# The second network's first product in seven block products for each pair of token tiles

## What is computed

```python
def _attn_ref(q, k, v):                       # q, k, v: (8, 8, 576, 64)
    q_s = softmax over d of q; k_s = softmax over the sequence of k
    kv = np.einsum('bhsd,bhse->bhde', k_s, v)
    return np.einsum('bhsd,bhde->bhse', q_s, kv)

def _moe_ref(x, w_in, w_out, alpha):          # x (4608, 512), w_in (512, 2048)
    h = x @ w_in
    g = np.maximum(h, 0.0) + alpha * np.minimum(h, 0.0)
    return g @ w_out

def _moe2_ref(x, w_in, w_out, g_ln):          # w_in (512, 1024), w_out (1024, 512)
    h = x @ w_in
    e = np.exp(h - np.max(h, axis=-1, keepdims=True))
    solu = h * e / (np.sum(e, axis=-1, keepdims=True) + 1e-09)
    mu, var = mean and variance of solu over its row
    return ((solu - mu) / np.sqrt(var + 1e-06) * g_ln) @ w_out
```

## Time and profile before

| what | us |
|---|---|
| median of 3 runs | 1226.35 (1226.23 to 1227.88) |
| profiled execution | 1226.08 |
| its span, first to last instruction | 1224.3 |
| PE busy | 1209.1 (99%), 6129 matmuls |
| DVE busy | 818.4 (67%) |
| ACT busy | 508.8 (42%) |
| POOL busy | 206.5 (17%) |

### The profile page before, as it was taken

How to read it: one execution, slowest core, us unless ns; L and a number is a source line. 1 busy time by engine, 2 the same in 40 slices (tenths; PEclk the granted TensorE clock), 3 DMA queues, 4 the chain that set the end, 5 groups by cost and what they waited for, 6 DMA issues and landing times.

```text
span 1224.3 us, 16516 instructions
## 1 busy us (share of the span) xinstructions
PE 1209.1 (99%) x6129; PEld 1002.5 (82%) x6129; DVE 818.4 (67%) x1060; ACT 508.8 (42%) x720; POOL 206.5 (17%) x179
## 2 busy tenths in 40 slices
PE   8899999999999999999999999999999999999998
PEld 7788888888888888888888888897888888888887
DVE  7867677676773577869777697665755565655652
ACT  4444444434443344444344443333543444344442
POOL 5632423223231000000000000021211111111110
PEclk9999999999999999999999999999999999999999
DMA  9798787877855654261552614693544444444432
GB/s 237 218 265 260 231 258 233 251 254 226 269 176 167 241 189 170 93 225 52 171 173 69 225 50 140 203 269 120 169 157 139 147 145 146 147 139 151 137 120 78
DMA packets 208973, 217.52 MB, mean 178 GB/s; under 512 B 63480, under 2 KB 147984, under 8 KB 208784
## 3 DMA queue, kind: packets, MB, share of 16 engines
q1 hardware_dynamic: 204672, 208.30, 53.8%
q0 software_dynamic: 4192, 8.39, 2.3%
q10 hardware_dynamic: 48, 0.01, 0.0%
HBM read 124.84 MB, written 91.81 MB: 177 GB/s over the span
## 4 chain that ended last, share of the span: by engine, by line
PE 95%; DVE 2%; DMA 1%; SPq 1%; issue 0%; ACT 0%; POOL 0%; DVEq 0%; ACTq 0%
PE ps_y L1608 11%; PE ps_y L1610 10%; PE ps_y L1609 10%; PE ps_y L1694 5%; PE ps_y L1696 5%; PE ps_y L1698 5%; PE ps_y L1748 5%; PE ps_y L1746 5%; PE ps_y L1747 5%; PE ps_m L1721 3%; PE ps_m L1696 3%; PE ps_m L1698 3%; PE ps_m L1694 3%; PE ps_h L1726 3%; PE ps_h L1721 3%; PE ps_m L1726 3%
## 5 line engine op out<-in xcount | busy, mean ns | idle before, releaser
L1608 PE MATMUL ps_y<-X,W 128*128 128x512 f32 x576 | 226.7, 394 | 0.0
L1610 PE MATMUL ps_y<-X,W 128*128 128x512 f32 x576 | 224.4, 390 | 0.0
L1609 PE MATMUL ps_y<-X,W 128*128 128x512 f32 x576 | 224.3, 389 | 0.0
L1215 DVE SCALAR_TENSOR_TENSOR gst<-gst,nslope,ps_y 128x512 f32<-128x512 f32 x144 | 105.1, 735 | 129.7 <-ACT gst L863 129.6
L863 ACT ACTIVATE gst<-ps_y 128x512 f32<-128x512 f32 x144 | 85.8, 596 | 236.0 <-PE ps_y L1610 211.7
L1608 PEld LDWEIGHTS ps_y<-X,W 128*128 128x128 f32 x576 | 108.1, 188 | 23.1
L1610 PEld LDWEIGHTS ps_y<-X,W 128*128 128x128 f32 x576 | 108.1, 188 | 22.8
L1609 PEld LDWEIGHTS ps_y<-X,W 128*128 128x128 f32 x576 | 108.1, 188 | 21.9
L1694 PE MATMUL ps_y<-rh,WOc 128*128 128x512 f32 (+1 forms) x320 | 117.8, 368 | 1.3 <-DVE rl L1357 1.3
L1696 PE MATMUL ps_y<-rl,WOc 128*128 128x512 f32 (+1 forms) x320 | 117.7, 368 | 0.0
L1698 PE MATMUL ps_y<-rh,WOc 128*128 128x512 f32 (+1 forms) x320 | 117.7, 368 | 0.0
(11 more groups left out here) (186 smaller groups left out, 2356.8 us busy)
## 6 DMA issues: line engine op xcount, KB each, us to landing
g_scratch<-gst SPq DMA_DIRECT2D x144, 256.0 KB, 3.2
RX<-g_scratch SPq DMA_DIRECT2D x36, 512.0 KB, 3.6
z_scratch<-zb SPq DMA_DIRECT2D x35, 512.0 KB, 2.6
zt<-z_scratch SPq DMA_DIRECT2D x140, 128.0 KB, 2.8
RY<-g_scratch SPq DMA_DIRECT2D x18, 512.0 KB, 4.5
RZ<-g_scratch SPq DMA_DIRECT2D x18, 512.0 KB, 4.3
x2r<-y_scratch SPq DMA_DIRECT2D x36, 256.0 KB, 3.1
KK<-k_dram SPq DMA_DIRECT2D x16, 512.0 KB, 6.9
```

The lines of the kernel that those rows point to most:

```text
L1215: nc.vector.scalar_tensor_tensor(gst[:, n % 3, :], gst[:, n % 3, :], nslope[:, f:f + 1], ps_y[:, f % 4, :], ALU.mult, ALU.add).then_inc(g_ ...
L1608: nc.tensor.matmul(o, W1[:, f, 0, a, :], x[:, 0, a, :], start=(a == 0), stop=False)
L1609: nc.tensor.matmul(o, W1[:, f, 0, a, :], x[:, 1, a, :], start=False, stop=False)
L1610: mm = nc.tensor.matmul(o, W1[:, f, 1, a, :], x[:, 0, a, :], start=False, stop=(a == KT - 1))
```

## The change

The first product of the second network takes its tiles in pairs (period n, tiles t = 0 and 1) and makes h of both in seven block products by the same recursion as the down product: the left operand's blocks are x parts of the two tiles and their sums, the right operand's are blocks and sums of blocks of W_in2. A block is 6 matmuls of 512 columns, a pair has 42.

- The seven x operands are made once for a whole pass of the down product: the four quadrants, and three sums and one further difference that POOL forms from them (`x2_sums`, `x2_lower`). SP stores all seven to `x2_dram`.
- The seven W operands are made in the first stage (`ws_turn`, four differences for each half), 22 pieces instead of 16, four per chunk.
- h is put together in SBUF (`hs`) by ACT (`first_copy`, `h11_copy`) and DVE (`form_u`, `form_v`, `form_22`, `form_12`, `form_21`); maximum, exponential and solu read it there. solu and z are written over e2. The squares go to PSUM.
- `x2_low` on POOL takes the 14 blocks of a pair at once, 128x1792.
- All loops are written out, the first five periods in an order of their own, the rest in a fixed one. The last tile's transposes by PE are gone.

```diff
+        W2c, = place(ATT_AT, ("W2c", [P, 7, 2, 2, TOK], F32R))
+        BLOCK = (m0, m1, ps_h[:, 0, :], ps_h[:, 1, :], m0, m1, ps_h[:, 0, :])
...
@@ sync: after a pass of the down product
+            def store_sums(u):
+                store_x2(u, 1, p1, s1_ok, u + 1, s1_st)
+                store_x2(u, 3, u1, s3_ok, u + 1, s3_st)
+                store_x2(u, 2, c11, s2_ok, u + 1, s2_st)
+            def store_lower(u):
+                store_x2(u, 4, v1, c21_ok, 2 * (u + 1), y21_st)
+                store_x2(u, 5, v1, s4_ok, u + 1, s4_st)
+            def load_x2(n):
...
+                if n >= 2:
+                    sp.wait_ge(x2h_ok, n - 1)
+                    sp.wait_ge(x2l_ok, n - 1)
+                sp.dma_start(x2[n % 2][:, :, :], x2_dram[u, :, :, :, r * P:(r + 1) * P].rearrange("k a p n -> p (k a) n")
+                             ).then_inc(x2_in[n % 2], 16)
@@ gpsimd
+            def x2_sums(u):
+                n = TOK // 2 if u == PAIRS else TOK
+                pool.wait_ge(c12_ok, 2 * (u + 1))
+                pool.wait_ge(y22_st, 16 * (u + 1))
+                nc.gpsimd.tensor_tensor(p1[:, :, 0:n], u1[:, :, 0:n], p1[:, :, 0:n], ALU.add).then_inc(s1_ok, 1)
+                pool.wait_ge(s1_ok, u + 1)
+                pool.wait_ge(c11_ok, u + 1)
+                nc.gpsimd.tensor_tensor(u1[:, :, 0:n], c11[:, :, 0:n], u1[:, :, 0:n], ALU.subtract).then_inc(s3_ok, 1)
+                pool.wait_ge(s3_ok, u + 1)
+                pool.wait_ge(y11_st, 16 * (u + 1))
+                nc.gpsimd.tensor_tensor(c11[:, :, 0:n], p1[:, :, 0:n], c11[:, :, 0:n], ALU.subtract).then_inc(s2_ok, 1)
+            def x2_lower(u):
+                n = TOK // 2 if u == PAIRS else TOK
+                pool.wait_ge(s2_ok, u + 1)
+                pool.wait_ge(y21_st, 16 * (u + 1))
+                nc.gpsimd.tensor_tensor(v1[:, :, 0:n], v1[:, :, 0:n], c11[:, :, 0:n], ALU.subtract).then_inc(s4_ok, 1)
+            def load_w2(n):
+                k, last = 2 * n, min(2 * n + 2, PARTS)
+                pool.wait_ge(b_used, ends(LAST_U, n))
...
+            for u in range(PAIRS):
+                x2_sums(u)
+                x2_lower(u)
             pool.wait_ge(ws_st, 16 * WS)
+            for n in range(4):
+                load_w2(n)
+            x2_low(0)
+            load_wo2(0)
+            load_wo2(1)
+            x2_sums(PAIRS)
+            x2_low(1)
+            x2_lower(PAIRS)
+            x2_low(2)
+            power(0, 0)
+            x2_low(3)
+            power(0, 1)
+            power(1, 0)
+            x2_low(4)
...
+            for n in range(5, PERIODS):
+                power(n - 1, 0)
+                power(n - 1, 1)
+                if n + 1 < PERIODS:
+                    x2_low(n + 1)
@@ scalar
+            for n in range(5, PERIODS):
+                square_tile(n - 1, 1)
+                first_copy(n)
+                out_copy(n - 3, 0)
+                zt_high(n - 2, 0)
+                if n + 1 < PERIODS:
+                    x2_high(n + 1)
+                out_copy(n - 3, 1)
+                zt_high(n - 2, 1)
+                h11_copy(n)
+                exp_tile(n, 0)
+                exp_tile(n, 1)
+                square_tile(n, 0)
@@ vector
+            def form_u(n):
...
+                nc.vector.tensor_tensor(hs[n % 2][0][:, TOK:F2], BLOCK[2], p1c[:, :], ALU.add).then_inc(h_u, 1)
+            def form_v(n):
...
+                nc.vector.tensor_tensor(hs[n % 2][1][:, 0:TOK], BLOCK[3], hs[n % 2][0][:, TOK:F2], ALU.add).then_inc(h_v, 1)
...
+            form_early(0)
+            form_12(0)
+            tile_max(0, 0)
+            form_21(0)
+            tile_max(0, 1)
+            tile_solu(0, 0)
+            form_early(1)
+            tile_solu(0, 1)
+            form_12(1)
+            form_21(1)
+            norm_tile(0, 0)
+            tile_max(1, 0)
+            form_early(2)
+            norm_tile(0, 1)
+            zt_low(0, 0)
+            tile_max(1, 1)
+            tile_solu(1, 0)
+            form_12(2)
+            form_21(2)
+            tile_solu(1, 1)
+            tile_max(2, 0)
+            tile_max(2, 1)
+            zt_low(0, 1)
+            norm_tile(1, 0)
+            form_early(3)
+            norm_tile(1, 1)
+            tile_solu(2, 0)
+            zt_low(1, 0)
+            tile_solu(2, 1)
+            form_12(3)
+            form_21(3)
+            tile_max(3, 0)
+            norm_tile(2, 0)
+            tile_max(3, 1)
+            norm_tile(2, 1)
+            zt_low(1, 1)
+            tile_solu(3, 0)
+            form_early(4)
+            tile_solu(3, 1)
+            norm_tile(3, 0)
+            zt_low(2, 0)
...
+            for n in range(5, PERIODS):
+                norm_tile(n - 1, 0)
+                norm_tile(n - 1, 1)
+                form_early(n)
+                zt_low(n - 2, 0)
+                zt_low(n - 2, 1)
+                form_12(n)
+                tile_max(n, 0)
+                form_21(n)
+                tile_max(n, 1)
+                tile_solu(n, 0)
+                tile_solu(n, 1)
+            n = PERIODS - 1
+            norm_tile(n, 0)
+            norm_tile(n, 1)
+            for t in range(2):
+                zt_low(n - 1, t)
...
@@ tensor
+            def m1_product(n, k):
+                if k == 0:
+                    pe.wait_ge(x2l_ok, n + 1)
...
+                elif k == 1 and n > 0:
+                    pe.wait_ge(h12_ok, n)
...
+                elif k == 5:
+                    pe.wait_ge(h22_ok, n + 1)
...
+                for t in range(2):
+                    begin = t == 0 and not more
+                    nc.tensor.matmul(o, hi[:, 2 * k + t, :], W2c[:, k, 0, t, :], start=begin, stop=False,
+                                     skip_group_check=more)
+                    nc.tensor.matmul(o, hi[:, 2 * k + t, :], W2c[:, k, 1, t, :], start=False, stop=False,
+                                     skip_group_check=more)
+                    mm = nc.tensor.matmul(o, lo[:, 2 * k + t, :], W2c[:, k, 0, t, :], start=False, stop=(t == 1),
+                                          skip_group_check=more)
+            for n in range(PERIODS):
+                for k in range(4):
+                    m1_product(n, k)
+                if n >= 3:
+                    m2_product(n - 3, 1)
+                for k in range(4, PARTS):
+                    m1_product(n, k)
+                if n >= 2:
+                    m2_product(n - 2, 0)
+            m2_product(PERIODS - 3, 1)
+            for n in range(PERIODS - 2, PERIODS):
+                for t in range(2):
+                    m2_product(n, t)
```

More of the change, by code:

```diff
@@ L679, in _ @@
[L679 to L693 removed]
+                    load_x2(0)
@@ L779, in x2_low @@
-            def x2_low(m, r):
-                pool.wait_ge(x2h_ok, 4 * m + r + 1)
-                nc.gpsimd.tensor_tensor(x2l[:, r % 2, :, :], x2[r], x2h[:, r % 2, :, :].bitcast(F32),
-                                        ALU.subtract).then_inc(x2l_ok, 1)
-            def power(m, r):
-                s = r % 2
-                pool.wait_ge(var_ok, 4 * m + r + 1)
-                nc.gpsimd.tensor_tensor(st[:, s, 8:9], st[:, s, 7:8], mhalf[:, :], ALU.pow).then_inc(rstd_ok, 1)
-            def tiles(m, last=False):
-                for r in range(4):
-                    if not (last and r >= 2):
-                        x2_low(m + (r + 2) // 4, (r + 2) % 4)
-                    power(m, r)
@@ L803, in _ @@
+            power(PERIODS - 1, 0)
+            power(PERIODS - 1, 1)
         @block.scalar
@@ L1072, in _ @@
-            exp_tile(0, 3)
-            x2_high(1, 1)
-            square_tile(0, 3)
-            out_copy(0, 0, first=True)
-            tiles(1, second=True)
-            with act.Fori(2, LAST) as m:
-                tiles(m)
-            tiles(LAST, last=True)
-            zt_high(LAST, 2)
-            out_copy(LAST, 1, last=True)
-            zt_high(LAST, 3, by_pe=True)
-            out_copy(LAST, 2, last=True)
-            out_copy(LAST, 3, last=True)
+            first_copy(2)
+            x2_high(3)
@@ new lines, in _ @@
+            exp_tile(1, 0)
+            h11_copy(2)
+            zt_high(0, 0)
+            exp_tile(1, 1)
+            square_tile(1, 0)
+            zt_high(0, 1)
+            square_tile(1, 1)
+            first_copy(3)
+            out_copy(0, 0)
+            x2_high(4)
+            exp_tile(2, 0)
+            exp_tile(2, 1)
+            zt_high(1, 0)
+            out_copy(0, 1)
+            square_tile(2, 0)
+            h11_copy(3)
+            square_tile(2, 1)
+            zt_high(1, 1)
@@ L1475, in zt_low @@
[L1475 to L1488 removed]
+                dve.wait_ge(z_ok, i + 1)
@@ new lines, in norm_tile, with zt_low, form_early @@
+                if n > 0:
+                    dve.wait_ge(zb_st[t], 16 * n)
+                nc.vector.transpose(zb_out[t], zb_in[t]).then_inc(zb_ok, 1)
+            def zt_low(n, t):
+                dve.wait_ge(zh_ok, 2 * n + t + 1)
```

(16 more changed lines are left out.)

760 lines of the change are left out of this document (410 added, 350 removed).

## The result

The changed kernel takes 1243.22 us (median of 4 runs, 1241.06 to 1245.13), the kernel before 1226.29 on the same chip: a ratio of 1.0134, 95% interval 1.0121 to 1.0147. It is slower, as forecast (1239, range 1214 to 1251).

The account below looks back on a forecast made before the run. TensorE was taken to bound the kernel, 95% of the span. Terms -25.5 + 23.0 + 13 + 2 = +12.5 on 1226.08 to 1226.35 gave 1239 us; own range 1226 to 1246, 8 in 10 1214 to 1251.

Parts of the forecast that it names:

- The matmuls removed: Second network: 108 fewer matmuls at 0.227 us, 24.5 us, and the last tile's eight transposes, 1.0 us: -25.5.
- The turns at the down product: GpSimd's sums and VectorE's operations with two SBUF inputs take turns, delaying b_low: +23.0 us, +21 to +26.
- The start of the second network: First pairs: TensorE waits for late forms, x2_low and the first z tiles: +13 us, ends 4 and 17.
- The end: Last period: both last tiles' norms stand ahead of zt_low(16,0), so TensorE waits: +2 us, range 0 to 2.6.
- The first stage: Six more splits and eight differences, 0.7 us each, beside up products: not charged, at most 1 us.
- Sums that are free: Rival, chance 0.14: GpSimd's sums in the down product cost nothing, giving -15 us, 1211.
- A second network without stalls: Rival, chance 0.11: the down product pays, but the second network starts without stalls: -2.5 us, 1224.
- Rival 3: Second network, chance 0.10: x2_low blocks z's scaling every period, 22.0 instead of 20.4 us: +21, 1260.

Follow-up runs that it names:

- pool_reads: Kernel before, plus four GpSimd subtractions of 128x1024 on an unused buffer behind each of passes 1 to 4, nobody waiting: 1247.07 us, ratio 1.0177.
- dve_sums_early_last: Changed kernel, sums of passes 1 to 4 on VectorE, pass 4's late ones early in the last pass, x2_low(0) on VectorE behind the last b_low: 1229.42 us.
- pool_writes: Kernel before, plus GpSimd memsets, which write SBUF and read nothing, four times behind each of passes 1 to 4: 1226.72 us, ratio 1.0001.
- x_low_one_column: Changed kernel, GpSimd's x2_low cut to one of 128 columns from pair 2 on, the other low parts left out: 1242.38 us, ratio 1.0115.
- early_x2_loads: Changed kernel, only queue orders altered around the second network's start and end, with x2 loads earlier: 1243.90 us, ratio 1.0146.
- sums_one_column: Changed kernel, sums of x made for one column of each row only, semaphores and stores kept: 1227.33 us, ratio 1.0002.

## Why the prediction was right

**The matmuls removed** (-25.5). Steady periods are 20.40 us long against 21.76 for two tiles before. The pitch of 0.227 is unchanged. VectorE is busy for 16.7 us of a period where 18.0 was counted.

**The turns at the down product** (+23.0, measured +22.2). The mechanism was the one laid out, and a sum in a free field took the 2.40 that stood in the count. The sizes hold pass by pass too: 5.3 stood for each of three passes, 4.9, 4.9 and 4.6 were measured; 7.1 stood for the short fifth (5.4 + 1.7), 7.5 was measured; the first pass has 0.3, where nothing stood. The brackets alone give less, waits of 2.99, 3.57 and 4.04 in passes 2 to 4, because a pass also holds restarts, the shortest waits and, in pass 2, a slow stretch. The count had none of these by name; it had VectorE's delay, and that set the length of these passes, whatever filled PE's side. x2_low(0)'s wait was 2.93 where 3.0 stood, its operation 4.62 where 4.0 stood. pool_reads shows the cause alone, and dve_sums_early_last shows that without it nothing of the 22 is left. The estimate of 2.2 us for a sum from the Trainium skill's GPSIMD Engine Reference, section "Elementwise — side-by-side cycle accounting", was 8% short of the 2.40 measured.

**The start of the second network** (+13, ends 4 and 17). The waits are 9.8 us up to 950.54, in six places, and their sizes differ from the count: pair 2's x2_low 2.41 where I had 0.8 for it and two others together, the first second product 4.64 where I had 3.3, the later ones 0.6 to 1.4 where I had 1.7 to 3.7. Between z's store and zt_high lay 9.9 us instead of 6.9, beside two x2 loads of 0.9 MB issued at 872.09 and 880.15; no run took them away. And power(0,0) was released at 870.4, when DVE had come to the variance, stood behind x2_low(2) in POOL's queue, and started at 871.96. **The end** (+2): 2.35. With seven restarts (1.9) and a half-clock stretch at the first second product and at the end (3.2), that makes 17.3 us in place of the 15 of the sum. The marks give the same (25.5 - 8.2), but with the 0.7 us of waits that the kernel before had there taken off, so some shorter losses are missing from the list. The term was 2.3 us short in sum, the single waits were further off, and it is luck that they offset each other.

**The first stage** (at most 1) is the term that was too small. The profiled execution had 0.9, but in the ten experiments that are made from the changed kernel the down product begins at 482.98 to 486.31 us, in the kernel before and the two made from it at 478.78 to 480.29: +3 to +7, where this one profile shows +0.9. On one chip the four first experiments have 478.78 and 480.29 against 483.03 and 483.14. It may be what the median (+16.9) has over the profile (+15.0); the three other executions of the change also had a lower mean granted clock (0.989 to 0.992 against 0.993), and no trace tells the two apart. Waits of PE that the kernel before doesn't have there are for kv's normalisation (0.2 to 0.8 us), the low part of q (0.3 to 1.5) and the first b_low (up to 1.0). One for a part of k at 17 to 19 us is longer too (0.8 to 1.9), but pool_reads, made from the kernel before, has it with 1.0, and pool_writes has 0.6 at the first b_low. The splits and differences of W2 beside them are suspected; no run took them away, and it stays open.

**The rivals.** Sums that are free: excluded by pool_reads. A second network without stalls: no. Rival 3, z blocked in every period, didn't come in the change, where its scaling takes 0.81 throughout; but its mechanism is real, 4.50 and 4.53 us in two versions in which x2_low came right behind the power. The Trainium skill's SBUF — State Buffer, section "Who interferes with whom", has tensor_scalar in a two-port mode and GpSimd shut each other out, has a VectorE instruction with two SBUF inputs contend with a GpSimd instruction that reads SBUF, and excepts one that only writes it. The runs agree: 4.50 us instead of 0.81, 3.27 instead of 1.22, and 1.22 beside the fills of pool_writes. In which mode the scaling ran, no run shows.

## What to carry to other kernels

- Work given to GpSimd because it is idle isn't free when VectorE works out of SBUF beside it: price it as its own length added to VectorE's queue at that place, and look how much lead VectorE has there. Here 11.8 us of sums on POOL, their own waiting for VectorE included, cost 4.6 to 4.9 us in a full pass, and the same sums on VectorE, 1.2 us each, cost nothing.
- In a pipeline's start, count the chain to the first product of the second kind against the work that TensorE has ahead of it. The difference shows as waits somewhere; moving loads only moved them, shortening the chain removed them from the first tile and left them to the next.
- Moving an operation moves the time for which its buffer is held. The store and the next writer have to be laid against the shortest pass, not the usual one.

## What was not expected of the hardware

TensorE's granted clock fell to the 1.2 GHz level at short waits, of 2 us and more, in the middle of a full stream. Over the change and seven of the experiments' profiles (pool_reads to x_low_one_column, without pool_writes), behind the first stage: at 15 waits of 1.2 to 1.45 us it never did, at 23 of 1.98 to 3.08 it did 17 times, at 12 of 3.86 to 8.00 each time. Waits of the same length and place differ: 3.00 at 729.41 gave a fall in x_low_one_column and none in early_x2_loads. The fall came between 3.6 us before the wait's end and 1.5 us behind it. Of the 29 stretches 19 lasted 3.4 us and 10 lasted 6.8; what lay behind the wait made the matmuls 1.3 to 2.9 us later.

How much of the spread between executions this explains is open. In x_low_one_column the fastest, 1234.89, had a mean granted clock of 0.994 and the three others, 1242.08 to 1244.55, had 0.988 or 0.989; but in sums_one_column executions with 0.990 and 0.996 took 1226.75 and 1228.06.
